# Attention, a routed expert stage and a dense ELU stage on one core: batches written out, a wider moving gate, routed rows turned one pair later, and two row maxima in another order

## The reference

```python
scores = scale * q @ k.T                      # causal mask, softmax
local = softmax(scores) @ v
q_p = where(q > 0, q, exp(q) - 1) + 1
mem_out = (q_p @ M_prev) / (q_p @ z_prev + 1e-6)
x = g * mem_out + (1 - g) * local             # g = sigmoid(beta), per head
x = x.transpose(0, 2, 1, 3).reshape(2304, 512)
logits = x @ w_gate                           # 8 experts, the largest wins
y[n] = gate_w[n] * (relu(x[n] @ w1[e]) @ w2[e])   # e = argmax(logits[n])
h = y @ w_in
out = where(h > 0, h, exp(min(h, 0)) - 1) @ w_out
```

## Time and profile before

| what | value |
|---|---|
| time, median of 3 runs | 1232.35 us (1223.26 to 1236.21) |
| the profiled execution's own time | 1237.84 us |
| its span | 1236.1 us |
| TensorE busy, share of the span | 1148.9 us, 93% |
| VectorE, ScalarE, GpSimd busy | 511.0, 334.2, 198.8 us |

### The profile page before, as it was taken

One profiled execution on the slowest core, in us unless ns is written; L12 is line 12 of the kernel. 1 busy time (PEld: TensorE's weight loads), 2 busy tenths in 40 slices (PEclk: granted clock), 3 DMA queues, 4 the chain that ended last, 5 costly groups with the idle time before them and its releaser, 6 DMA issues.

```text
span 1236.1 us, 20700 instructions
## 1 busy us (share of the span) xinstructions
PE 1148.9 (93%) x6988; PEld 971.4 (79%) x6989; DVE 511.0 (41%) x968; ACT 334.2 (27%) x533; POOL 198.8 (16%) x134
## 2 busy tenths in 40 slices
PE   6998997899999978998998999789999999999998
PEld 4777786677778866787886887579998999989997
DVE  4355235316331434536226326444343343434332
ACT  2222212213121202334215215332222322222222
POOL 0001112112210222316005105430000000000000
PEclk9999577859555969999999999889999999999999
DMA  3113114111410218627106415420000000100000
GB/s 81 31 51 109 31 32 141 32 31 51 141 31 11 78 46 255 246 78 261 51 34 203 153 34 170 148 73 27 26 26 1 25 25 25 25 26 1 26 1 26
DMA packets 57679, 88.53 MB, mean 72 GB/s; under 512 B 30608, under 2 KB 30608, under 8 KB 57616
## 3 DMA queue, kind: packets, MB, share of 16 engines
q1 hardware_dynamic: 47808, 65.35, 16.9%
q10 hardware_dynamic: 6768, 12.32, 3.0%
q0 software_dynamic: 3040, 9.96, 2.5%
HBM read 67.68 MB, written 19.94 MB: 71 GB/s over the span
## 4 chain that ended last, share of the span: by engine, by line
PE 67%; issue 20%; POOL 6%; DVE 3%; DMA 2%; ACT 1%; ACTq 1%; SPq 0%; POOLq 0%; DVEq 0%
PE ps L809 17%; PE ps L822 16%; PE ps L609 10%; PE ps L517 7%; POOL wparts L403 5%; PE ps L584 2%; PE ps L630 2%; PE ps L530 2%; PE ps L487 2%; PE ps L761 2%; PE ps L475 2%; PE ps L467 1%; PE ps L617 1%; DVE negmax L1131 1%; PE ps L478 1%
## 5 line engine op out<-in xcount | busy, mean ns | idle before, releaser
L809 PE MATMUL ps<-th,wparts 128*128 128x384 f32 x768 | 198.5, 339 | 4.5 <-ACT orow L1047 3.0
L822 PE MATMUL ps<-wparts,gh 128*128 128x512 f32 x576 | 179.4, 392 | 0.0
L809 PEld LDWEIGHTS ps<-th,wparts 128*128 128x128 f32 x768 | 142.3, 190 | 12.9 <-issue 3.8
L609 PE MATMUL ps<-vbuf,probT 128*128 128x65 f32 (+1 forms) x896 | 131.1, 303 | 0.0
L809 PE MATMUL ps<-tl,wparts 128*128 128x384 f32 x384 | 130.3, 339 | 0.0
L738 PE MATMUL ps<-wparts,xh 128*128 x368 | 118.0, 402 | 12.4 <-DVE xl L1311 9.6
L609 PEld LDWEIGHTS ps<-vbuf,probT 128*128 128x128 f32 (+1 forms) x896 | 118.8, 214 | 5.1
L761 PE MATMUL ps<-wparts,hh 128*128 x352 | 113.7, 405 | 8.4 <-POOL wparts L403 2.8
L822 PEld LDWEIGHTS ps<-wparts,gh 128*128 128x128 f32 x576 | 106.6, 188 | 18.3
L822 PE MATMUL ps<-wparts,gl 128*128 128x512 f32 x288 | 113.7, 395 | 0.0
L403 POOL TENSOR_TENSOR wparts<-stage,wparts 128x1024 fp32r<-128x1024 f32 (+1 forms) x32 | 88.0, 2762 | 127.2 <-ACT wparts L872 126.8
(11 more groups left out here) (187 smaller groups left out, 1674.1 us busy)
## 6 DMA issues: line engine op xcount, KB each, us to landing
stage<-weights SPq DMA_DIRECT2D x52, 512.0 KB, 4.9
stage_first<-weights SPq DMA_DIRECT2D x28, 512.0 KB, 5.4
xs<-x_sorted ACTq DMA_DIRECT2D x24, 256.0 KB, 2.7
y_slots<-yrow ACTq DMA_DIRECT2D x23, 256.0 KB, 2.1
kraw<-kT SPq DMA_DIRECT2D x16, 288.0 KB, 3.0
qraw<-qT SPq DMA_DIRECT2D x16, 288.0 KB, 3.3
out<-orow SPq DMA_DIRECT2D x18, 256.0 KB, 2.1
vbuf<-v_main SPq DMA_DIRECT2D x32, 128.0 KB, 2.4
```

The source lines that it names most:

```text
L609: mm = nc.tensor.matmul(weighed(h)[0:rows, i, :], p, v, start=j == 0, stop=j == i)
L809: mm = nc.tensor.matmul(ps[:, H_B[f % 2], 0:GN], wparts[:, at:at + P], x[:, r, c, :], start=c == 0 and x is th and part == 0, stop=c == DC ...
L822: mm = nc.tensor.matmul(ps[:, j, :], x[:, f % RING, P * j:P * j + P], wparts[:, at:at + D], start=f == 0 and x is gh and part == 0, stop=f ...
```

## The change

- Each engine's loop over batches becomes a Python loop: four batches of straight code, with constants in the waits. `wait_alone` becomes a plain wait nearly everywhere, and `link` counts on.
- The moving operand of a logits product is the gate repeated twelve times side by side (96 columns instead of 8). Only the first 8 columns of a result are read; the next tile's result is written over the others. The place moves from bank 6 to bank 7, where `weigh` of head 1 also writes, so that pairs 2 and 3 wait for the copies of logits and ranks ahead of `weigh(*last, 1, ...)`.
- Tiles 0 and 1 are turned in pair 1 behind `unit` 0, tiles 2 and 3 behind `weigh(*last, 1, (0, 1))`, tile 4 behind `unit` 1. In that pair `maxima` steps 0 and 1 move behind, the latter after `unit` 2, and the logits follow it. ScalarE's copies and its `weights_high` of that pair move with them.
- In all other pairs `maxima` step 2 is put ahead of `weigh(*last, 1, (3, 4))`, right behind `unit` 2, and VectorE's `row_max` 2 ahead of `attention_part` of head 1. The copy of the logits moves from `attention_part` of head 0 to that of head 1 of the pair before.

```diff
 
-        LG, PFX, TOT = (B_OUT, FREE + TAIL), (B_OUT + 1, FREE), (B_OUT + 1, FREE + QT * E)
+        LG, PFX, TOT = (B_OUT + 1, FREE), (B_OUT + 1, FREE), (B_OUT + 1, FREE + QT * E)
+        COPIES = (BANK - FREE - QT * E + E) // E
...
 
             def logits(b, i):
-                wait_alone(pe, xt_copied, b * QT + i + 1)
+
+                pe.wait_ge(xt_copied, b * QT + i + 1)
                 rows = P if i < QT - 1 else TAIL
+                out = ps[0:rows, LG[0], LG[1] + E * i:LG[1] + E * (i + COPIES)].rearrange("p (n e) -> p n e", e=E)
                 for c in range(DC):
-                    mm = nc.tensor.matmul(small(LG)[0:rows, i, :], xT[:, i, c * rows:(c + 1) * rows],
-                                          wg[:, c, :], start=c == 0, stop=c == DC - 1)
+                    mm = nc.tensor.matmul(out, xT[:, i, c * rows:(c + 1) * rows],
+                                          wg[:, c, :].unsqueeze(1).to_broadcast([P, COPIES, E]),
+                                          start=c == 0, stop=c == DC - 1)
                 mm.then_inc(lg_done, 1)
 
             def ranks(b):
 
-                wait_alone(pe, hot, b + 1)
+                pe.wait_ge(hot, b + 1)
                 nc.tensor.matmul(ps[:, PFX[0], PFX[1]:PFX[1] + QT * E], before[:], onehot[:].rearrange("p i e -> p (i e)"),
                                  start=True, stop=True)
...
                 last = (b if m else b - 1, (m - 1) % PB)
+                routing = prev and m == 1
                 unit(b, m, 0, prev)
-                if prev and m == 1:
-                    wait_alone(pe, xt_copied, (b - 1) * QT + 2)
-                    turn_pair(b - 1, (2, 3))
+                if routing:
+                    pe.wait_ge(memx_done, b * PB + 2)
+                    turn_pair(b - 1, (0, 1))
                 unit_tail(b, m, prev)
                 if older:
-                    if prev and m == PB - 1:
-                        wait_alone(pe, rank_copied, b)
+                    if prev and m in (2, 3):
+                        pe.wait_ge(lg_copied if m == 2 else rank_copied, b)
                     weigh(*last, 1, (0, 1), last[1] > 0 or prev)
-                if prev and m == 1:
-                    wait_alone(pe, xt_copied, (b - 1) * QT + 4)
-                    turn_pair(b - 1, (4,))
-                    wait_alone(pe, xt_copied, b * QT)
-                if behind:
+                if routing:
+                    pe.wait_ge(xt_copied, (b - 1) * QT + 2)
+                    turn_pair(b - 1, (2, 3))
+                elif behind:
                     maxima(b, m + 1, 0)
                 unit(b, m, 1, prev)
+                if routing:
+                    pe.wait_ge(xt_copied, (b - 1) * QT + 4)
+                    turn_pair(b - 1, (4,))
                 if older:
                     weigh(*last, 1, (2,), prev)
-                if behind:
+                if routing:
+                    pe.wait_ge(xt_copied, b * QT)
+                    maxima(b, m + 1, 0)
+                elif behind:
                     maxima(b, m + 1, 1)
                 unit(b, m, 2, prev)
+                if behind:
+                    maxima(b, m + 1, 1 if routing else 2)
+                if routing:
+                    for i in range(QT):
+                        logits(b - 1, i)
                 if older:
                     if prev and m == 2:
                         ranks(b - 1)
                     weigh(*last, 1, (3, 4), prev)
-                if behind:
+                if routing:
                     maxima(b, m + 1, 2)
                 weigh(b, m, 0, (0, 1), prev)
                 if behind:
                     maxima(b, m + 1, 3)
-                weigh(b, m, 0, (2, 3), prev)
-                if prev and m == 1:
-                    for i in range(QT):
-                        logits(b - 1, i)
-                weigh(b, m, 0, (4,), prev)
+                weigh(b, m, 0, (2, 3, 4), prev)
                 if behind:
                     memory(b, m + 1)
-                if prev and m == 0:
-                    wait_alone(pe, memx_done, b * PB + 2)
-                    turn_pair(b - 1, (0, 1))
...
-            batch(0, False, True)
-            with pe.Fori(1, B - 1) as b:
-                batch(b, True, True)
-            batch(B - 1, True, False)
+            for b in range(B):
+                batch(b, b > 0, b < B - 1)
...
                     softmax(b, m, 0, prev)
                     if prev and m == 1:
-                        for i in (2, 3):
+                        for i in (0, 1):
                             copy_routed(b - 1, i, B_MAX + i % 2)
                     softmax_tail(b, m)
                     if prev and m == 1:
-                        copy_routed(b - 1, 4, B_MAX)
-                    if prev:
+                        for i in (2, 3):
+                            copy_routed(b - 1, i, B_MAX + i % 2)
+                    elif prev:
                         weights_high(m, (b - 1) * (2 * MATRIX), b * 16, 0)
                     softmax(b, m, 1, prev)
+                    if prev and m == 1:
+                        copy_routed(b - 1, 4, B_MAX)
+                        weights_high(m, (b - 1) * (2 * MATRIX), b * 16, 0)
                     if prev and m == 2:
                         exp_routed(b - 1)
                     softmax(b, m, 2, prev)
                     if m + 2 < PB or more:
                         parts_high(b, m + 2, True)
-                    if prev and m == 0:
-                        for i in (0, 1):
-                            copy_routed(b - 1, i, B_MAX + i % 2)
...
                         row_max(b, m + 1, 0)
                         query_low(b, m + 1)
                         row_max(b, m + 1, 1)
+                        if not (prev and m == 1):
+                            row_max(b, m + 1, 2)
                     if older:
-                        attention_part(b if m else b - 1, (m - 1) % PB, 1, prev)
+                        attention_part(b if m else b - 1, (m - 1) % PB, 1, prev, b - 1 if prev and m == 1 else None)
                     if prev and m == 2:
                         copy_ranks(b - 1)
                     if behind:
-                        row_max(b, m + 1, 2)
+                        if prev and m == 1:
+                            row_max(b, m + 1, 2)
                         row_max(b, m + 1, 3)
                     if prev and m == 0:
                         for i in range(QT):
@@ -1237,7 +1239,7 @@
                         count_tiles(b - 1)
                         place(b - 1)
                         gate(b - 1)
-                    attention_part(b, m, 0, prev, b - 1 if prev and m == 1 else None)
+                    attention_part(b, m, 0, prev)
                     if behind:
                         memory_part(b, m + 1, prev)
```

More of the change, by code:

```diff
@@ L283, in load_values @@
                 if free:
-                    wait_alone(sp, pv_done, pair * 2 - 2)
+                    sp.wait_ge(pv_done, pair * 2 - 2)
                 for h in range(2):
@@ L429, in _ @@
             pool.wait_ge(made, 14)
-            batch(0, False)
-            with pool.Fori(1, B) as b:
-                batch(b, True)
+            for b in range(B):
+                batch(b, b > 0)
             for h in range(2):
@@ L500, in maxima @@
                 if step == 0:
-                    wait_alone(pe, k_hi, pair + 1)
-                    wait_alone(pe, q_hi, pair + 1)
-                    if m or not isinstance(b, int) or b:
-                        wait_alone(pe, memx_done, pair)
+                    pe.wait_ge(k_hi, pair + 1)
+                    pe.wait_ge(q_hi, pair + 1)
+                    if pair:
+                        pe.wait_ge(memx_done, pair)
                 else:
-                    wait_alone(pe, max_done, pair * STEPS + step)
+                    pe.wait_ge(max_done, pair * STEPS + step)
                 if step < STEPS - 1:
@@ L554, in unit @@
                 else:
-                    wait_alone(pe, p_done, pair * UNITS + 1)
+                    pe.wait_ge(p_done, pair * UNITS + 1)
                     mm = block(columns(0, 2 * P), m, 2, 2 * P, MAIN)
@@ L929, in _ @@
             parts_high(0, 1, False)
-            batch(0, False, True)
-            with act.Fori(1, B - 1) as b:
-                batch(b, True, True)
-            batch(B - 1, True, False)
+            for b in range(B):
+                batch(b, b > 0, b < B - 1)
             for i in range(QT):
@@ L1064, in link @@
                 seen[0] += 1
-                dve.wait_ge(own, seen[1] + seen[0])
+                dve.wait_ge(own, seen[0])
             nc.vector.memset(vbuf[:, :, :, :, HD:], 1.0).then_inc(zeroed, 1)
@@ L1250, in _ @@
             memory_part(0, 0, False)
-            batch(0, False, True)
-            before_loop += seen[0]
-            with dve.Fori(1, B - 1) as b:
-                seen[0], seen[1] = 0, (b - 1) * OWN + before_loop
-                batch(b, True, True)
-                assert seen[0] == OWN, (seen, OWN)
```

(4 more changed lines are left out.)

52 lines of the change are left out of this document (24 added, 28 removed).

## The result

The changed kernel took 1158.42 us, the median of 4 runs (1151.34 to 1171.7), the kernel before 1229.49 on the same chip (4 runs, 1223.26 to 1236.21): ratio 0.9402, 95% interval 0.9315 to 0.9489. Run once more beside the last experiments, on another chip, it took 1180.88 against 1223.45, ratio 0.9654 (0.9573 to 0.9736). It is faster by 3 to 6%; the forecast of 1150 was 8 us low in the first comparison, and the second median lies 31 us above it, 0.9 us outside its range (1122 to 1180). Ratios given with an interval are of undisturbed runs alone; medians are of all runs.

What follows compares the result with a forecast made beforehand. TensorE, busy nearly all the span, was taken to be bound by its clock. From 1237.84, 81 (97 at full clock, less 12 and 4 for falls) and 3 at the stage's end give 1154, taken as 1150; range 1122 to 1180.

Steps and rivals of the forecast that it cites:

- The sum at full clock: Fifteen pairs from 45.22 to 438.40 with TensorE at full clock throughout: 296 us, 97 less than 393.18.
- copies' wait: In the routed pair, TensorE waits for ScalarE's fifth copy of turned rows, behind softmax 1: 0.55 us, 1.1 before.
- memx wait: TensorE's wait for memx before the first turned tiles: 2.2 us when exposed, unit 0 covers 1.54, leaving 0.66.
- The maxima's exchange: Score step 2 and row_max 2 earlier in 11 ordinary pairs save 0.97 us each, 10.7, and the fall behind goes.
- Falls in the routed pair: Half clock behind the three routed pairs' remaining waits: 12 us up to the logits, 4 behind the 1.2 us wait.
- What is late next: nothing within 1 us at full clock: In ordinary pairs after the maxima change places, no other result comes late for TensorE within 1 us.
- I am wrong if ordinary pairs show half clock: Sign against the forecast in the changed profile; ordinary pairs were expected to take 17.8 us at clock 1.00.
- Full clock throughout: Rival: the two waits left in the routed pair don't make the clock fall; 1137 us, chance 0.20.
- Wide logits that don't bring the clock back: Rival: routed pairs stay at half clock until the next pair's unit 0, 39 us in all; 1180 us, chance 0.16.
- Transposes as idle: Rival: the routed pair's clock falls at the first turn, 7 us become 12; 1164 us, chance 0.09.
- Half clock that runs on: Rival: clock doesn't return in unit 0, so thirteen pairs lose 14 us each; 1320 us with all at half, chance 0.05.
- A stop of 8 us in straight code: Rival: code loading stops the written-out batches one or two times, 8 us each; inside the range, no chance given.

Runs made afterwards that it cites:

- number 1: The changed kernel with VectorE's choose and choose_first of pair 2 moved behind row_max 0: 1130.86 us, ratio 0.92.
- number 5: number 1 with the exchange of the two maxima undone in ordinary pairs: 1186.09 us.
- number 3: The changed kernel with one copy of the gate (8 columns) in place of twelve: 1168.46 us, ratio 0.9525.
- number 4: The kernel before with its batches written out and nothing else changed: 1222.77 us, ratio 0.9877.
- number 11: number 1 with turned rows, score step 2, row_max 2 and copies reordered to remove the routed pair's waits; this repeat took 1143.69 us, ratio 0.9338.
- number 9: The changed kernel with GpSimd's weights_low in pair 2 made to wait for VectorE's choose: 1137.45 us, ratio 0.9357.
- number 7: number 1 with the gate standing once (8 columns) in place of twelve times (96): 1172.64 us, ratio 0.968.
- number 2: The changed kernel with GpSimd's weights_low of pair 2 moved from behind add_memory h=0 to behind h=1: 1168.01 us, ratio 0.9394.
- number 10: The changed kernel with only the second half of the choose (three small instructions) moved behind row_max 0: 1191.6 us, one run.
- number 12: The changed kernel itself, unedited, run again on the third chip: 1180.88 us, ratio 0.9654.

## Why the prediction was right, and where it was off

**The sum at full clock** was 296 us for fifteen pairs, 294.5 to the point where the 329.52 end. Measured: 329.52, less 30.6 for pair 2 (83.67 us for three in place of 3 x 17.7), 3.8 for the half clock that ran on into pairs 3 (19.02, 18.63 and 17.79 where number 1's take 17.62, 17.62 and 16.44), 6.2 in batch 2's routed pair: 289. Number 1's trace, with one short fall, has 294.0. Its terms: first of the fifteen 19.1, measured 17.62, since the clock was up already (19.17 in number 1); ordinary pair 17.82, measured 17.62; routed pair 26.9, measured 25.97 where nothing fell; forty wide logits 4.4, measured 4.50; twenty transposes 0.11 each, measured the same (8 in about 1 us from 295.0); copies' wait 0.55, measured 0.2; memx wait 0.66, measured 0.2, 1.6 and 0.7; row_max 2 in the routed pair 1.2, measured 0.99. The back edge's 7.8 us went, and longer code cost nothing.

**The maxima's exchange** was right in kind and mis-sized in worth: 10.7 us in the sum "and the fall behind this wait goes with it"; number 5 puts it at 34 to 55, most of it clock.

**Falls in the routed pair** were priced at 12 + 4 us over the three pairs. One of three fell and cost 4.7 of clock. It fell at 207.4, 1.2 us behind the copies' wait, as foretold, but that wait was only 0.2 long, and 7.7 us before the fall a memx wait of 1.6 had ended. Number 1 has waits of 2.2 and 0.2 at the same two places and didn't fall there, so which of them counts isn't shown. It rose at 217.7, inside the wide logits, as foretold. Waits of 0.2 and 0.99 left the others up.

**The step that failed**, though the time fell in the range, is "What is late next: nothing within 1 us at full clock". I asked that of attention_part and of softmax 1, not of what pair 2 has alone, the choose. Pair 2 had always begun at half clock, where such a delay hardly counts (two of number 3's three), and where GpSimd's piece began after the choose had ended (172.10, choose's product at 171.13 to 171.33). With pair 2 at full clock, both begin within 0.1 us of each other in every batch. That cost 34 us. Pairs 2 are ordinary pairs in my sum, ten at 17.82, so that "I am wrong if ordinary pairs show half clock" came true in three of them. The rule was there to be read: the Trainium skill, "SBUF — State Buffer", Who interferes with whom, says that a VectorE instruction with two SBUF inputs contends with a GpSimd instruction that reads SBUF, that the order of issue decides which of the two is blocked, and that on this chip reductions never contend. The traces agree in every case above: 0.20 to 2.38 us, 0.75 to 2.97, GpSimd's 2.41 to 3.02, and the reductions unchanged.

**Why 1150 was still near.** Largely by luck. Against the 34 us stand the first pair's early rise, 9.3 us; 5 by which the sum at full clock was too high, 1.5 of them from the same rise; 10 by which falls in the routed pairs were priced too dear; and 4.7 at the end of the stage where I took 3. On the other chip, where the changed kernel took 1180.88, they didn't suffice. The early rise isn't the change's: in 10 of the 14 traces the clock's records begin at full clock between 22.0 and 28.3 us, in four (before, numbers 1, 4 and 11) near 48, and the order of work ahead of it is the same in all.

**The rivals.** Full clock throughout (1137): not the changed kernel, but close to number 9's 1137 and number 1's 1131, for another reason than I gave. Wide logits that don't bring the clock back: wrong, by the rise at 217.7, by the eight rises behind the last pair and by number 7 against number 1. Transposes as idle, by the rule in Part 4 of the Trainium skill's "TensorE: Matmul & The Clock Gate": not here, since routed pairs with twenty transposes ran at clock 1.00 from end to end (106.43 to 132.40 and 292.57 to 319.12). Half clock that runs on: not in the first trace, but the form that it takes is real, in numbers 2 and 5 and in the changed kernel's second trace (31.4 us for a pair 3 behind a fallen pair 2). A stop of 8 us in straight code: none seen in the stage.

## What to carry to other kernels

When a stage speeds up, look again at every pair of engines whose work used to be apart by half a microsecond: ask of each VectorE instruction ahead of a result that TensorE waits for whether it reads two SBUF operands while GpSimd works, and put it behind that result, or let GpSimd wait for it. Read the min and max of a line's duration, not its mean or median: a blocked instruction is counted as busy and no view of waits names it. And price a wait of TensorE above its length when it can lower the clock: here an exchange that saved 11 us of waits was worth 34 us or more.

## What the runs showed besides

On the third chip all four kernels (numbers 9 to 12) show one event that the other chips' traces don't have at that place: at the start of batch 2, and in numbers 9 and 11 of batch 3 too, VectorE and ScalarE both start on TensorE's memory products 1.8 to 4.1 us behind the start of the last of them, where it is 0.3 to 0.5 us otherwise. VectorE's and ScalarE's lines in number 12 (the products ended by 174.5):

```profile
176.77 0.17 DVE L1141 TENSOR_SCALAR minv<-ps 128x10 f32<-128x10 f32 x1 [2.53 <-remote]
```

```profile
176.82 0.68 ACT L892 ACTIVATE qphi<-qraw 128x576 f32<-128x576 f32 x1 [8.22 <-remote]
```

In five of these six places the clock fell within 7 us of the pair's start (in number 9 at 256.8); in number 12 that pair 0 took 29.47 us, 17.63 in the first trace of the same kernel. The weights' burst and the scatter begin there, but no run varied them, so the cause stays open.
